# Second layer of a two-scale attention and MoE kernel: output units in two runs of six a step, products in rows of four and three

## The reference

```python
def _moe2_ref(x, w_in, w_out):          # x (2304, 512), w_in (512, 2048), w_out (2048, 512)
    h = x @ w_in
    g = h * np.cos(h)
    return (g @ w_out).astype(np.float32)
```

## Time and profile before

| | us |
|---|---|
| median of 3 runs | 689.71 |
| lowest, highest | 689.37, 691.17 |
| the profiled execution | 691.25 |
| its span in the profile | 689.5 |
| PE busy in it | 676.2 |

### The profile page before, as it was taken

The page is one execution under the profiler, slowest core; times in us unless marked ns, Lnnn a source line. Parts: engine busy times, 40 slices in busy tenths (PEclk is TensorE's granted clock), DMA queues, the critical chain, the costliest instruction groups (busy, mean ns, idle before and its releaser), DMA issues.

```text
span 689.5 us, 12757 instructions
## 1 busy us (share of the span) xinstructions
PE 676.2 (98%) x4763; PEld 599.8 (87%) x4767; DVE 445.4 (65%) x814; ACT 407.8 (59%) x849; POOL 233.1 (34%) x315
## 2 busy tenths in 40 slices
PE   7899999999999999999999999999999999999998
PEld 4677789889889899999898988889888988988986
DVE  7798975664662333367888888965555676655553
ACT  4668875655564656475666657654445675545444
POOL 6897854553523555401222245600000430000000
PEclk9999999999999999999999999999999999999999
DMA  9954231321100000556543252432222336322202
GB/s 291 298 171 140 85 118 39 125 89 67 36 1 1 1 1 1 183 218 246 181 165 138 108 214 107 168 139 107 108 107 106 129 142 242 116 107 106 107 1 91
DMA packets 18445, 82.77 MB, mean 120 GB/s; under 512 B 1872, under 2 KB 5968, under 8 KB 15056
## 3 DMA queue, kind: packets, MB, share of 16 engines
q1 hardware_dynamic: 18384, 81.96, 34.3%
HBM read 62.56 MB, written 19.40 MB: 119 GB/s over the span
## 4 chain that ended last, share of the span: by engine, by line
PE 90%; DVE 4%; POOL 2%; issue 2%; DMA 1%; ACT 1%; SPq 0%; POOLq 0%; ACTq 0%; DVEq 0%
PE ps L1601 28%; PE ps L1578 25%; PE ps L1465 15%; PE ps L1434 13%; PE ps L1449 2%; PE ps L1406 1%; PE ps L1356 1%; PE ps L1344 1%; PE ps L1392 1%; DMA qk_in<-in_qk 1%; PE ps L1381 1%; PE ps L1366 1%; DVE turn L1279 1%; DVE soft L1085 0%; DVE whole L1276 0%
## 5 line engine op out<-in xcount | busy, mean ns | idle before, releaser
L1578 PE MATMUL ps<-y_parts,w_parts 128*128 128x384 f32 x1008 | 203.2, 336 | 0.7 <-ACT part L949 0.7
L1578 PEld LDWEIGHTS ps<-y_parts,w_parts 128*128 128x128 f32 x1008 | 180.4, 188 | 15.8 <-ACT part L949 1.1
L1601 PE MATMUL ps<-wo,g_hi 128*128 128x512 f32 x576 | 179.2, 392 | 0.0
L1601 PEld LDWEIGHTS ps<-wo,g_hi 128*128 128x128 f32 x576 | 105.8, 188 | 11.8
L1601 PE MATMUL ps<-wo,g_lo 128*128 128x512 f32 x288 | 114.3, 397 | 0.0
L963 ACT ACTIVATE turn<-h,quarter 128x384 f32<-128x384 f32 x96 | 59.0, 615 | 79.6 <-DVE h L1271 79.4
L1465 PE MATMUL ps<-ln_hi,w_split 128*128 128x384 f32 x384 | 103.2, 339 | 0.0
L1285 DVE TENSOR_TENSOR turn<-h,turn 128x384 f32<-128x384 f32 x96 | 61.7, 642 | 43.9 <-ACT turn L969 43.9
L1271 DVE TENSOR_TENSOR h<-ps,part 128x384 f32<-128x384 f32 x72 | 40.1, 557 | 56.9 <-PE ps L1578 56.8
L1434 PE MATMUL ps<-w_split,x_hi 128*128 128x512 f32 x288 | 73.0, 395 | 0.7 <-DVE xT L1140 0.6
L609 POOL TENSOR_TENSOR y_parts<-xT,y_parts 128x768 fp32r<-128x768 f32 x17 | 32.8, 1944 | 117.5 <-ACT y_parts L834 117.5
(11 more groups left out here) (113 smaller groups left out, 972.7 us busy)
## 6 DMA issues: line engine op xcount, KB each, us to landing
w_parts<-w_kept SPq DMA_DIRECT2D x16, 1792.0 KB, 7.4
w_kept<-w_parts SPq DMA_DIRECT2D x8, 1792.0 KB, 6.7
qk_in<-in_qk SPq DMA_DIRECT2D x16, 586.0 KB, 4.4
vblk<-in_v_blocks SPq DMA_DIRECT2D x16, 384.0 KB, 5.6
v<-in_v_rows SPq DMA_DIRECT2D x16, 288.0 KB
result<-o_sb SPq DMA_DIRECT2D x18, 256.0 KB, 3.6
xT<-in_w_in SPq DMA_DIRECT2D x8, 512.0 KB, 7.8
raw_wo<-in_w_out SPq DMA_DIRECT2D x8, 512.0 KB, 6.7
```

The source lines that it names most:

```text
L1578: last = nc.tensor.matmul(product_ps(s, k), w[:, m, a, c, :], y_parts[:, n, b, c, :], start=(not adds and c == 0 and m == 0 and n == 0), s ...
L1601: last = nc.tensor.matmul(o_ps(tile), g[n][:, t * P:(t + 1) * P], wo[:, p, w, f, :], start=(first and m == 0), stop=(done and m == 2))
```

## The change

`UNITS` goes from (2, 2, 1, 2, 2, 1, 2) to (0, 0, 6, 0, 0, 6, 0). PE then runs P1, P2, P6, six units, P5, P7, P3, six units, P4, and P4 is followed at once by the next step's P1, P2, P6. The number of products and units is the same, and each unit keeps its place among the units. ACT's and DVE's loops are rewritten: every operation is still there, once, and the semaphores that it waits for are the same. The points that the prediction speaks of: on ACT `copy_corner(s)` moves from the end of step s to the start of step s + 1, behind `cosine(s, 1)`; `split_y` of T3 and B22 moves from the first step of a pass to the last of the one before; `split_g(s - 1, 2)` and `(s - 1, 3)` stand between the copies of P6 and P5. On DVE `split_w(s + 1, True)` moves from ahead of `times_cos(s, 0)` to behind `fraction(s, 1)`. The order of POOL and SP is unchanged. The diff, cut to its core:

```diff
-UNITS = (2, 2, 1, 2, 2, 1, 2)
+UNITS = (0, 0, 6, 0, 0, 6, 0)
...
             for s in range(STEPS):
                 q, j = s // JOINS, s % JOINS
+
+                if s:
+                    copy_corner(s - 1)
+                if s == 1:
+                    copy_x2(GROUPS - 1, 3)
+                if s:
+                    to_turns(s - 1, 3)
+                copy_part(s, P1)
+                if s:
+                    cosine(s - 1, 2)
+                    split_g(s - 1, 1)
+                if s + 1 < JOINS:
+                    split_w(s + 1, False)
                 if j == 1 and q:
                     copy_out(q - 1, 2)
+                if j == 0 and q:
+                    split_y(q, T4)
                 if s:
-                    to_turns(s - 1, 3)
-                    cosine(s - 1, 2)
-                copy_part(s, P1)
...
                     cosine(s - 1, 3)
...
+                if j == JOINS - 1 and q + 1 < PASSES:
+                    split_y(q + 1, B11)
                 copy_part(s, P6)
                 if s == 0:
                     copy_x2(GROUPS - 1, 1)
+
+                to_turns(s, 0)
+                if s:
+                    split_g(s - 1, 2)
+                    split_g(s - 1, 3)
+                if j == JOINS - 1 and q + 1 < PASSES:
+                    split_y(q + 1, B21)
+                if j == 1 and q:
+                    copy_out(q - 1, 3)
+
+                copy_part(s, P5)
+                cosine(s, 0)
+                if j == 1 and q:
+                    copy_out(q - 1, 4)
+                    copy_out(q - 1, 5)
+                if j == JOINS - 1 and q + 1 < PASSES:
+                    split_y(q + 1, T2)
                 if s + 1 < JOINS:
                     split_w(s + 1, True)
...
                 if j == JOINS - 1 and q + 1 < PASSES:
-                    split_y(q + 1, T1)
+                    split_y(q + 1, T3)
                 to_turns(s, 2)
-                copy_corner(s)
+                cosine(s, 1)
                 if j == 0 and q:
                     copy_out(q - 1, 0)
                     copy_out(q - 1, 1)
-                cosine(s, 1)
-                if s == 0:
-                    copy_x2(GROUPS - 1, 3)
+                if j == JOINS - 1 and q + 1 < PASSES:
+                    split_y(q + 1, B22)
...
                 if s:
                     times_cos(s - 1, 1)
                     fraction(s - 1, 3)
-                    times_cos(s - 1, 2)
-                    split_g(s - 1, 1)
                 add_corner(s, 0)
                 if s:
+                    split_g(s - 1, 1)
+                    times_cos(s - 1, 2)
                     times_cos(s - 1, 3)
+                fraction(s, 0)
+                if s + 1 < JOINS:
+                    split_w(s + 1, False)
+                if s:
                     split_g(s - 1, 2)
-                fraction(s, 0)
+                times_cos(s, 0)
                 if s:
                     split_g(s - 1, 3)
-                if s + 1 < JOINS:
-                    split_w(s + 1, False)
-                    split_w(s + 1, True)
-                times_cos(s, 0)
                 add_corner(s, 1)
                 split_g(s, 0)
+                add_corner(s, 2)
+                fraction(s, 1)
+                if s + 1 < JOINS:
+                    split_w(s + 1, True)
                 if 2 <= s <= 5:
                     split_wo(s + 2)
-                add_corner(s, 2)
-                fraction(s, 1)
                 fraction(s, 2)
```

More of the change, by code:

```diff
@@ L1005, in _ @@
                 q, j = s // JOINS, s % JOINS
+                if s:
[10 more added lines that the diff above has]
+                    split_w(s + 1, False)
                 if j == 1 and q:
                     copy_out(q - 1, 2)
+                if j == 0 and q:
+                    split_y(q, T4)
                 if s:
-                    to_turns(s - 1, 3)
-                    cosine(s - 1, 2)
-                copy_part(s, P1)
-                if j == 1 and q:
-                    copy_out(q - 1, 3)
-                if s:
-                    split_g(s - 1, 1)
-                    cosine(s - 1, 3)
-                if s + 1 < JOINS:
-                    split_w(s + 1, False)
[L1019 to L1027, removed]
+                    cosine(s - 1, 3)
+                if j == JOINS - 1 and q + 1 < PASSES:
+                    split_y(q + 1, B11)
                 copy_part(s, P6)
@@ L1030, in _ @@
                     copy_x2(GROUPS - 1, 1)
+                to_turns(s, 0)
[13 more added lines that the diff above has]
+                    split_y(q + 1, T2)
                 if s + 1 < JOINS:
                     split_w(s + 1, True)
-                if q and j == 0:
-                    split_y(q, B22)
+                split_g(s, 0)
                 if j == JOINS - 1 and q + 1 < PASSES:
[L1036 to L1048, removed]
+                    split_y(q + 1, T1)
                 to_turns(s, 1)
@@ L1051, in _ @@
                     copy_x2(GROUPS - 1, 2)
+                if 2 <= s <= 5:
+                    split_wo(s + 2)
                 if j == JOINS - 1 and q + 1 < PASSES:
-                    split_y(q + 1, T1)
+                    split_y(q + 1, T3)
                 to_turns(s, 2)
-                copy_corner(s)
+                cosine(s, 1)
                 if j == 0 and q:
@@ L1058, in _ @@
                     copy_out(q - 1, 1)
-                cosine(s, 1)
-                if s == 0:
-                    copy_x2(GROUPS - 1, 3)
+                if j == JOINS - 1 and q + 1 < PASSES:
+                    split_y(q + 1, B22)
             s = STEPS - 1
+            copy_corner(s)
             to_turns(s, 3)
@@ L1323, in _ @@
             fraction(s, 3)
+            split_g(s, 1)
             times_cos(s, 2)
-            split_g(s, 1)
             times_cos(s, 3)
```

## The result

| | before | after |
|---|---|---|
| median | 690.44 us (4 runs) | 697.45 us (4 runs) |
| lowest, highest | 689.37, 691.46 | 697.05, 697.64 |
| profiled execution, its span | 691.25, 689.5 | 697.05, 695.3 |

The ratio is 1.010, with a 95% interval of 1.0088 to 1.0112: the change makes the kernel 1.0% slower. The forecast was 696.3 us. Against the larger sets of runs of the kernel before that the experiments have beside them (medians 689.9 and 690.1) the loss is 7.3 to 7.6 us.

A forecast was written before the change was run, and what follows sets the result against it. PE, through the spacing of its matmuls, was taken as the bound. Waits of 10.2 us (1.1 of old waits already taken off) less 3.65 gained made it 6.6 us slower: 696.3 us, range 690.5 to 701.

The forecast's parts named there:

- The bound, the gain: PE's matmul spacing sets a step; grouping cuts it from 15.69 to 15.53 us, 3.65 us less in all.
- 0.01 for the products behind the runs: Extra time in a new step for products that follow runs of six units, 0.01 us.
- The three waits at nothing: P2, P6 and P3 in ordinary steps: about 0.13 us to spare, so no cost; other end 10 us.
- Rival C: The rows of products stall in every step, 10 us on top: 703 to 707 us; 7%.
- Rival A: The gain alone, as DVE catches up within its spare: 685 to 686 us; 12%.
- step 7: Step 6 to 7: POOL's make_y delays four DVE operations by 6.3 us, and PE loses 2.3 us.
- P2 of step 8: Step 7 to 8: P2 waits 3.8 us, as at step 15 to 16 but with DVE 2 us later.
- P2 of step 16: Step 15 to 16: P2 waits 1.8 us for copy_corner behind DVE operations delayed by POOL's splits.
- before's waits: The old kernel's PE waits at make_y of the third pass, 1.1 us, go away.
- so clock is no term: Granted clock is 1.00, the level of 2.4 GHz, so it adds nothing to the forecast.
- the row for step 8 to 9: make_y of the third pass delays DVE: P3 waits 1.8 us and corner 3's units 1.6, 3.4 new.
- Rival D: The skill's gap by columns holds: no gain from runs of six, same waits, 700 us; 5%.
- Rival B: Only the worst handoffs stall, 3 to 4 us, a sum near zero: 688.5 to 691.5 us; 9%.

The follow-up runs named there:

- e2: The changed kernel with POOL's make_y and split_y of passes 2 and 3 on 16 of 384 columns of tokens, the rest left out: 686.23 us.
- e3: The kernel before with POOL's make_y and split_y of passes 2 and 3 on 16 of 384 columns of tokens, the rest left out: 689.03 us.
- e1: The kernel before with the new UNITS alone, ACT's and DVE's old orders kept: 707.57 us.
- e10: The kernel before with the third pass's make_y spread over steps 10 to 13, nothing else: 688.86 us.
- e4: The changed kernel with copy_corner(s) put back ahead of cosine(s, 1) in steps 7 and 15 alone: 696.26 us.
- e5: The changed kernel with POOL's four make_y of the third pass started one a step in steps 10 to 13: 696.13 us.
- e8: e2 with small copies on ACT ahead of copy_corner, 20 at the start of step 12 and 28 at the start of step 18: 693.26 us.
- e9: The kernel before with the changed orders of ACT and DVE, the old UNITS kept: 702.82 us.
- e6: e5 with cosine(s, 1) of steps 7 and 15 and the split of B22 moved on ACT behind the next step's copy of P1: 690.03 us.

## Why the prediction was right

**The bound, the gain.** PE bound as said (the PEld of the page, 87%, which the prediction passes over, are PE's own weight loads), and a step became shorter by the spacing of its matmuls. The size was off: 15.57 and not 15.53. The term that failed is "0.01 for the products behind the runs". PE's timeline of after, in step 2:

```profile
335.08 3.31 PE L1586 MATMUL ps<-y_parts,w_parts 128*128 128x384 f32 x18
338.22 0.63 PE L1609 MATMUL ps<-wo,g_hi 128*128 128x512 f32 x2
```

Eighteen matmuls take 3.14 us where three products at 1.04 take 3.12. I had taken over the 1.045 of a product behind two units; behind a run of six the next product takes 1.06, as it does behind one unit, twice in a step. The gain is 2.6 us by the steps, 2.8 by e2 and e3, against 3.65. The 4.12 us for a run of six was right.

**The three waits at nothing.** Right: in none of the ordinary steps does PE wait, and e1 shows how near it is, with two more operations on ACT costing 0.5 us a step. Rival C (every step stalls) is out.

**DVE late, and what stands behind it.** Right in mechanism and place: e2 takes all waits away by POOL's work alone, which rules out that the orders wait by themselves. Rival A, that DVE catches up within its spare, is out by the waits of after. PE's idle time went to `copy_corner` as foretold, 5.6 us in two waits; for `part` it was 1.6 us where 3.5 were forecast, for `g_lo` 1.4 where 2 were. In step 7 the four DVE operations that were to lie under the burst do, at 404.30, 406.29, 408.42 and 410.45, and lose 6.3 us together, as said. In size: step 7 2.2 (forecast 2.3), P2 of step 8 3.5 (3.8), P2 of step 16 1.9 (1.8), before's waits 1.1 (1.1; e10).

**What was wrong.** The prediction's sentence "so clock is no term" failed: around P2's wait in step 8 the clock fell, and 17 slow matmuls behind it cost 2.8 us. And the row for step 8 to 9, 3.4 us, came to 0.7, all of it at corner 3's units: P3 didn't wait. The two belong together. ACT, DVE and PE of after in that step:

```profile
437.15 0.53 ACT L980 ACTIVATE g_hi<-turn 128x384 fp32r<-128x384 f32 x1 [1.60 <-DVE turn L1291]
438.30 0.49 ACT L949 ACTIVATE part<-ps 128x384 f32<-128x384 f32 x1 [0.62 <-PE ps L1586]
```

```profile
442.23 0.55 DVE L1296 TENSOR_TENSOR g_lo<-turn,g_hi 128x384 fp32r<-128x384 f32 x1
```

```profile
442.84 0.74 PE L1609 MATMUL ps<-wo,g_hi 128*128 128x512 f32 x2 [0.41 <-DVE g_lo L1296]
```

The copy of P5 (438.30) did stand behind `split_g(7, 3)` on ACT, as forecast, but ACT was then free 0.62 us before PE, which ran 2.8 us late by its lower clock. DVE works with hardly any idle time from 428.67 until its own `split_g(7, 3)` ends at 442.78, and corner 3's unit starts 0.06 behind that. So the slow matmuls filled time in which PE would have waited. At full clock P3 would have waited about 2.2 us and the units 1.3 (an estimate: 2.8 - 0.62, and 0.7 + 0.62), near the 1.8 and 1.6 forecast, and step 8 would have lost the same 7.0 us, where 3.8 + 3.4 = 7.2 were forecast. Two things fit this. In e4 the matmuls are slow only until 431.6 (433.9 in after), and there P3 waits 0.3 us and the units 1.6. And in the other three executions of after the mean clock is 0.997 to 0.998, so less time was spent at the lower level than in the profiled one (0.995), but their spans are no shorter (695.5 to 695.8 against 695.3). No run has the burst of step 8 without the lower clock, so it isn't shown by an experiment. Where no later wait takes the slow matmuls up they do cost: 1.6 us in e5, 2.7 in e8. That the missed clock term did so little harm to the forecast (696.3, measured 697.45) is luck: a burst that happened to follow took it up.

**Rival D**, that runs of six give nothing, is out: e2 is 2.8 us under e3. Rival B (a sum near zero) is out by the interval.

## What to carry to other kernels

When the bound engine leaves no idle time, ask of a new order not only whether the engines behind it have time on average, but what each handoff has to spare, and put that against the longest delay that a shared resource can bring (here POOL's operations, each of which holds DVE for up to 1.7 us, three or four in a row). A tight order can be used in the steps that are quiet, and a loose one kept where the bursts are; the bursts themselves can often be spread. Undoing the line that the longest wait names may only move the wait to the next one in the list.

## What the runs showed of the hardware

- A long pause of PE can cost more than itself. In after, e1, e4, e5, e8 and e9 the granted clock fell to half (1.2 GHz) around a wait of 3.2 to 4.0 us for weights, and matmuls of 128x384 then came every 0.32 us instead of 0.17 until it rose; this cost 2.7 us in e8 and 1.6 in e5. In e9 it also fell around a wait of 2.3 us. It didn't around P2's wait of 2.2 us in step 8 of e9, nor around the waits of 2.0 us and less in after, e6 and e8. The Trainium skill (TensorE: Matmul & The Clock Gate, What's actually happening) has the clock depend on how busy PE has been, and these runs agree.
- While POOL works through operations of 128x768, an operation of DVE that reads SBUF takes up to 1.7 us longer: in after a subtraction 2.04 us for 0.56, and `TENSOR_SCALAR`, which has one input, 2.00 for 0.35. A sum that reads one input from PSUM keeps its 0.54.
- A matmul's distance to the next depends on its neighbours: three of 128x512 take 0.70 us behind a product and 0.68 deep in a run, and a product takes 1.04 us behind another, 1.045 behind two units and 1.06 behind one or six. Why two units leave the least trace isn't settled.
